# Attention split by queries and its result kept on chip, in a fused attention and feed-forward kernel

## The reference, cut to what matters

```python
# q, k, v: (4, 8, 576, 64), block-causal mask with blocks of 64
scores = q @ k.transpose(0, 1, 3, 2) / sqrt(64)
scores = where(pos_i // 64 >= pos_j // 64, scores, -1e9)
attn = exp(scores - max); attn = attn / (attn.sum(-1) + 1e-9)
x = (attn @ v).transpose(0, 2, 1, 3).reshape(2304, 512)
h = x @ moe_w_in                      # 512 x 2048
g = where(h >= 1, h, where(h <= -1, 0, (h + 1) ** 2 / 4))
x = g @ moe_w_out                     # 2048 x 512
h = x @ moe2_w_in
out = (h * cos(h)) @ moe2_w_out
```

## Time and profile before

| | |
|---|---|
| median of 3 runs | 1106.37 us (1103.53 to 1107.26) |
| span of the profiled execution | 1103.5 us, which is also its time |
| TensorE busy | 1036.5 us, 94% |
| VectorE, ScalarE, POOL busy | 683.7 (62%), 571.5 (52%), 392.7 us (36%) |
| mean granted clock of TensorE | 0.975 |
| first feed-forward matmul | 119.7 us |
| first layer's outputs copied at | 198.9, 272.9, 347.0, 419.6, 492.1, 555.3, 601.4, 647.5 us, ... |
| second layer, one tile | 45.4 us |

### The profile page before, as it was taken

How to read it: one execution, slowest core, us unless ns; L and a number is a source line. 1 busy time by engine, 2 the same in 40 slices (tenths; PEclk the granted TensorE clock), 3 DMA queues, 4 the chain that set the end, 5 groups by cost and what they waited for, 6 DMA issues and landing times.

```text
span 1103.5 us, 21274 instructions
## 1 busy us (share of the span) xinstructions
PE 1036.5 (94%) x7424; PEld 972.7 (88%) x7424; DVE 683.7 (62%) x1308; ACT 571.5 (52%) x1166; POOL 392.7 (36%) x382
## 2 busy tenths in 40 slices
PE   5767899998998999989999999999999999999997
PEld 4646799898998998989999999899999999999996
DVE  6888666767677667676322248755555655556553
ACT  6877565555555655555333236554444444544443
POOL 5877453444353534443221222221222222222221
PEclk8887999999999999999999999999999999999999
DMA  4453212121221121221021025210101101011000
GB/s 152 146 186 125 86 55 71 52 65 65 67 79 56 58 64 61 63 69 41 26 78 38 0 77 176 93 32 7 38 0 38 38 0 38 0 38 38 0 20 20
DMA packets 28513, 64.93 MB, mean 59 GB/s; under 512 B 2880, under 2 KB 11584, under 8 KB 28480
## 3 DMA queue, kind: packets, MB, share of 16 engines
q1 hardware_dynamic: 28480, 64.50, 18.1%
HBM read 50.33 MB, written 14.16 MB: 58 GB/s over the span
## 4 chain that ended last, share of the span: by engine, by line
PE 78%; DVE 9%; ACT 6%; issue 6%; DMA 0%; DVEq 0%; POOL 0%; ACTq 0%; POOLq 0%
PE hidden L1042 35%; PE acc L1061 17%; PE acc L1068 14%; PE heads_out L972 4%; DVE q_parts L699 3%; PE turned L957 2%; PE scores L941 2%; PE scores L942 2%; DVE neg_max L710 2%; ACT probs L495 2%; ACT k_hi L485 1%; ACT q_parts L488 1%; ACT pt_hi L500 1%; DVE pt_lo L726 1%; ACT work L602 1%
## 5 line engine op out<-in xcount | busy, mean ns | idle before, releaser
L441 POOL TENSOR_TENSOR g_lo<-work,g_hi 128x512 fp32r<-128x512 f32 x144 | 189.4, 1315 | 445.6 <-ACT g_hi L608 445.5
L1042 PE MATMUL hidden<-x_hi,win_hi 128*128 128x256 f32 x1152 | 331.0, 287 | 0.8 <-DVE work L849 0.4
L1042 PE MATMUL hidden<-x_lo,win_hi 128*128 128x256 f32 x1152 | 326.9, 284 | 0.0
L1042 PE MATMUL hidden<-x_hi,win_lo 128*128 128x256 f32 x1152 | 325.6, 283 | 0.0
L1042 PEld LDWEIGHTS hidden<-x_hi,win_hi 128*128 128x128 f32 x1152 | 217.7, 189 | 6.0 <-DVE work L849 0.9
L1042 PEld LDWEIGHTS hidden<-x_lo,win_hi 128*128 128x128 f32 x1152 | 218.6, 190 | 2.9
L1042 PEld LDWEIGHTS hidden<-x_hi,win_lo 128*128 128x128 f32 x1152 | 220.1, 191 | 0.0
L399 POOL TENSOR_SCALAR probs<-probs,row_inv 128x512 f32<-128x512 f32 (+4 forms) x130 | 91.2, 708 | 214.2 <-DVE row_inv L722 214.2
L1068 PE MATMUL acc<-g_hi,wout_hi 128*128 128x256 f32 x576 | 166.0, 288 | 0.0
L1068 PE MATMUL acc<-g_hi,wout_lo 128*128 128x256 f32 x576 | 162.3, 282 | 0.0
L1068 PE MATMUL acc<-g_lo,wout_hi 128*128 128x256 f32 x576 | 162.2, 282 | 0.0
(11 more groups left out here) (97 smaller groups left out, 1939.0 us busy)
## 6 DMA issues: line engine op xcount, KB each, us to landing
qk_raw<-qk SPq DMA_DIRECT2D x32, 576.0 KB, 3.7
x_raw<-x_scratch SPq DMA_DIRECT2D x18, 512.0 KB, 3.9
v_raw<-v SPq DMA_DIRECT2D x32, 160.0 KB, 3.5
x_scratch<-out_work SPq DMA_DIRECT2D x32, 144.0 KB, 2.3
x_scratch<-y_stage SPq DMA_DIRECT2D x9, 512.0 KB, 2.7
out<-y_stage SPq DMA_DIRECT2D x9, 512.0 KB, 3.0
x_raw<-w_in SPq DMA_DIRECT2D x8, 512.0 KB, 5.5
y_stage<-w_out SPq DMA_DIRECT2D x8, 512.0 KB, 5.9
```

What stands on the lines that cost most here:

```text
L441: nc.gpsimd.tensor_tensor(g_lo[:, m % G_RING, :], work[:, m % 2, :], g_hi[:, m % G_RING, :], ALU.subtract).then_inc(g_lo_made, 1)
L1042: last = nc.tensor.matmul(into, w[:, p, c, half * P:(half + 1) * P], x[:, c, :], start=(i == 0), stop=(i == len(products) - 1))
```

## The change

A head becomes two items. Items 0 to 31 are the early ones: rows 0 to 255 of a head, two tiles, 256 keys. Items 32 to 63 are the late ones: rows 256 to 575, three tiles, 576 keys. Tokens are reordered so that the early rows of all batches come first: token tile `t` then needs only the first `TILE_ITEMS[t]` items, tile 0 eight of them. Nine early items run alone, with four weight pieces split beside them; the other twelve are split in tile 0 (`weights_beside`), and 264 slots (three per early item, six per late one) are spread over tiles 0 to 6: 24 over 20 units and 9 over 12 in tile 0, 41 over 32 units in tiles 1 to 5, 26 over 20 in tile 6. Sums of the two v parts go straight into a ring of three token tiles on chip (`x_raw`, `X_RING`), `add_parts`; the DRAM scratch and its loads are gone. All attention code is unrolled. ScalarE copies and stores a first-layer tile itself (`store_acc`), and the final output goes out in four DMAs of 64 rows per tile. The padding of narrow matmuls to 192 columns is dropped. Before, k and q came in one load of 576 KB per head; now early items have a load of half the size or less, double-buffered, and late ones one buffer.

```diff
+EARLY, LATE = 256, S - 256
+ITEMS = 2 * HEADS
+SLOTS_OF = (3, 6)
+TILE_ITEMS = [8, 16, 24, 32, 40, 48, 56, 64, 64]
+QUEUE = [(n, k) for n in range(H + 1, ITEMS) for k in range(SLOTS_OF[late(n)])]
+QUEUE += [(ITEMS, k) for k in range(3)]
+PER_TILE = [[(24, 20), (9, 12)]] + [[(41, 32)]] * 5 + [[(26, 20)]]
+WEIGHTS_ALONE = {1: (0, 0), 3: (0, 1), 5: (1, 0), 6: (0, 2)}
...
 # POOL
+            def attention(n, k):
+                if n == ITEMS:
+                    return
+                if k == 0 and not late(n):
+                    split_k(n + 1)
+                if k == 1:
+                    normalise(n, tiles_of(n)[0])
+                    normalise(n, tiles_of(n)[1])
+                if k == 2:
+                    split_v(n)
+                if k == 4:
+                    normalise(n, 4)
+                    if n + 1 < ITEMS:
+                        split_k(n + 1)
...
 # ScalarE
+            def attention(n, k):
                 if k == 0:
+                    if n < ITEMS:
+                        if not late(n):
+                            split_hi(n + 1)
+                        exponential(n, tiles_of(n)[0])
+                        exponential(n, tiles_of(n)[1])
+                    if n:
+                        turned_hi(n - 1, 2 if late(n - 1) else 0)
                 if k == 2:
+                    if n:
+                        move_part(n - 1)
+                    if n < ITEMS:
+                        split_v(n)
+                        if late(n):
+                            turned_hi(n, 0)
                 if k == 3:
                     turned_hi(n, 1)
                     exponential(n, 4)
+                if k == 4 and n + 1 < ITEMS:
+                    split_hi(n + 1)
...
+            def store_acc(t):
                 act.wait_ge(g_used, G_RING + PAIRS * (t + 1))
                 act.wait_ge(y_stored, 16 * (t + 1))
...
                 nc.scalar.activation(y_stage[:, :], acc[:, :, :].rearrange("p a n -> p (a n)"),
                                      ACT.Copy).then_inc(acc_read, 1)
+                act.wait_ge(acc_read, t + 2)
+                nc.scalar.dma_start(x2_dram[t, :, :], y_stage[:, :]).then_inc(y_stored, 16)
...
 # VectorE
+            def attention(n, k):
                 if k == 0:
+                    if n < ITEMS:
+                        row_max(n, tiles_of(n)[0])
+                        row_max(n, tiles_of(n)[1])
+                        if not late(n):
+                            split_q(n + 1)
+                    if n:
+                        turned_lo(n - 1, 2 if late(n - 1) else 0)
+                if k == 1 and n < ITEMS:
+                    inverse(n, tiles_of(n)[0], 2)
                 if k == 2:
+                    if n:
+                        add_parts(n - 1)
+                    if n < ITEMS and late(n):
+                        turned_lo(n, 0)
                 if k == 3:
                     turned_lo(n, 1)
+                    row_max(n, 4)
                 if k == 4:
                     inverse(n, 4)
+                    if n + 1 < ITEMS:
+                        split_q(n + 1)
...
 # TensorE
+            def weigh(n):
+                pe.wait_ge(pt_lo_made, first_turn(n) + (3 if late(n) else 1))
+                pe.wait_ge(v_lo_made, n + 1)
+                if n:
+                    pe.wait_ge(heads_read, n)
+                if late(n):
+                    width = LATE
+                    parts = [(j, LATE * j, max(P * j - EARLY, 0)) for j in range(5)]
+                else:
+                    width = EARLY
+                    parts = [(0, 0, 0), (1, P, P)]
...
             def attention(n, k):
                 if k == 0:
+                    if n < ITEMS:
+                        score(n, tiles_of(n)[0])
+                        score(n, tiles_of(n)[1])
+                    if n:
+                        turn(n - 1, 2 if late(n - 1) else 0)
                 if k == 2:
+                    if n:
+                        weigh(n - 1)
+                    if n < ITEMS and late(n):
+                        turn(n, 0)
                 if k == 3:
                     turn(n, 1)
                     score(n, 4)
```

More of the change, by code:

```diff
@@ L209, in probs_chunk @@
[L209 to L215, removed]
-        def probs_tile(i, alone):
-            whole = probs_chunk(i, alone, 0, EXT[i])
-            return whole.rearrange("p (a n) -> p a n", a=2) if i == QT - 1 else whole
-        def turned_bank(i, alone):
-            return scores[:, 1, :] if alone and i % 2 else turned
@@ L343, in _ @@
-            with sp.Fori(0, 5) as t:
-                beside_tile(t, BESIDE, False)
-            beside_tile(5, HEADS - HEADS_A - BESIDE * 5, True)
+                sp.dma_start(x2_dram[t, :, :], y_stage[:, :]).then_inc(y_stored, 16)
+            load_qk(0)
+            load_first(0, 0)
+            load_v(0)
+            load_qk(1)
+            load_v(1)
+            load_first(1, 0)
+            sp.sem_inc(y_stored, 16)
+            for n in range(ITEMS):
+                after_split(n)
+                for which, pair in FIRST_AFTER.get(n, ()):
+                    load_first(which, pair)
+                if n:
+                    after_split_v(n - 1)
@@ L452, in tile @@
                         hidden_lo(t, s + LAG)
+                    if beside:
+                        for n, k in beside[u]:
+                            attention(n, k)
+                        w = weights_beside(t, u)
+                        if w and w[0] == 1:
+                            split_wout(w[1])
                     s = made_in.get(u)
@@ new lines, in add_parts @@
+            def add_parts(n):
+                dve.wait_ge(part_moved, n + 1)
+                pieces = list(x_pieces(n))
+                for first, cols, place, tile in pieces:
+                    if tile >= X_RING:
+                        dve.wait_ge(x_lo_made, 2 * (tile - X_RING + 1))
+                    last = nc.vector.tensor_tensor(place, heads_out[half_rows(n), first:first + cols],
+                                                   part_sum[half_rows(n), first:first + cols], ALU.add)
+                last.then_inc(heads_read, 1)
@@ L903, in _ @@
             split_q(0)
-            attention_alone(0, True, first=True)
-            with dve.Fori(1, PAIRS) as n:
-                attention_alone(n, True)
-            for n in range(PAIRS, HEADS_A):
-                attention_alone(n, False)
-            split_x(0)
-            end_alone()
+            for n in range(H + 1):
+                for k in range(3):
+                    attention(n, k)
+                w = WEIGHTS_ALONE.get(n)
+                if w and w[0] == 0:
+                    split_win(w[1])
+            split_x(0, False)
             for m in range(LAG):
@@ new lines, in weigh @@
+            def weigh(n):
+                pe.wait_ge(pt_lo_made, first_turn(n) + (3 if late(n) else 1))
+                pe.wait_ge(v_lo_made, n + 1)
+                if n:
+                    pe.wait_ge(heads_read, n)
+                if late(n):
+                    width = LATE
+                    parts = [(j, LATE * j, max(P * j - EARLY, 0)) for j in range(5)]
+                else:
+                    width = EARLY
+                    parts = [(0, 0, 0), (1, P, P)]
+                for j, at, first in parts:
+                    for buf in (pt_hi, pt_lo):
+                        last = nc.tensor.matmul(heads_out[:, first:width], v_parts[:, j, :, :].rearrange("p a d -> p (a d)"),
+                                                buf[:, at + first:at + width], start=(j == 0 and buf is pt_hi),
+                                                stop=(j == parts[-1][0] and buf is pt_lo))
```

848 lines of the change are left out of this document (345 added, 503 removed).

## The result

The changed kernel takes 1265.09 us (median of 4 runs, 1256.34 to 1268.77) where the kernel before takes 1106.82 (1103.53 to 1107.73): 1.143 times as long, 95% interval 1.139 to 1.147. The forecast was slower, 1209 us in a range of 1140 to 1270. The measured time lies in that range, near its upper end.

What follows compares the result with a forecast made beforehand. It took the chain between late items' scores, with TensorE waiting, as the bound: 55 + 8 (lead-in) + 73 + 68 + 464 + 12.5 + 22.7 + 502.1 + 1 = 1206, plus 0.3% gives 1209 us; range 1140 to 1270.

Steps and rivals of the forecast that it cites:

- The alone phase: Attention before any feed-forward work: first hidden matmul at 55 us against 119.7, a gain of 65 us.
- The rival by which TensorE sets the pace (1085): Elementwise engines keep up, late items cost TensorE's own 10.95 us each, total 1085 us; chance 0.11.
- narrow matmuls: 192 unpadded matmuls in attention, taken at 0.11 us each; the upper end adds at most 31 us.
- the term of the late items: Late items beside feed-forward: 32 at 14.5 us, a 14.1 us chain from split_q to split_q plus 0.4, together 464 us.
- the tiles' ends: The x split and store_acc add 2.5 us per tile, 12.5 us together.
- either way the loop's sum differs little: Late items: whether split_q waits for one POOL instruction or more hardly matters, since k_lo is itself the chain's next-to-last link.
- a rival of its own (1240 to 1270, 0.12): TensorE's clock falls in the late stage, adding 1 to 2 us per item: 1240 to 1270 us; chance 0.12.
- a sign that would prove it wrong: A late stage with TensorE's clock under 0.9 would prove the forecast wrong.
- the likeliest case (1150 to 1240): The forecast itself: a late-item loop of 13 to 15.5 us, total 1150 to 1240 us; chance 0.67.
- tile 0: Eleven early items beside feed-forward, eight sharing ScalarE and VectorE with ten weight splits: 73 us.
- tile 1: First 28 units with twelve early items at 5.5 us each, plus 2 for the x split: 68 us.
- the rest of tile 6: After its last slots, 14 units at 20.2 us plus 2.5 for closing turn and weighing: 22.7 us.

Runs made afterwards that it cites:

- e2: Changed kernel with a late item's last score, maximum and exponential moved to slot 2, its inverse, normalise and the next item's splits to slot 3: 1165.66 us.
- e1: Changed kernel with POOL waiting for split_q behind split_k in slot 4: 1255.43 us.
- e13: e4 with turn(n, 1) and its two copies in slot 4 in place of slot 3: 1136.87 us.
- e11: e4 with the output-weight splits beside tile 0 one unit earlier: 1153.57 us.
- b1: The kernel before, with POOL waiting for split_q behind split_k in slot 6: 1086.72 us.
- e7: e4 with turn(n, 1) and its copies one slot later, weigh(n - 1) and move_part(n - 1) one slot earlier: 1197.68 us.
- e9: e4 with SP's wait for v_lo(n - 1) and load of v ahead of tile 0's weight loads: 1154.53 us.
- e3: Changed kernel with split_k(n + 1) ahead of normalise(n, 4) in POOL's slot 4: 1220.49 us.
- e8: e7 with turn(n, 2) and its copies in the item's own slot 5, not the next item's slot 0: 1178.27 us.
- e4: e2 with the next item's splits ahead of the turned copies in slot 3, and e1's wait on POOL: 1152.52 us.

## Why the prediction was right, and where it was off

**Right: the mechanism.** TensorE waits in each late item for the chain that ends in `split_k`, `split_q`. e2 shows it: the same instructions with the chain started a slot earlier give back 99 of the 158 us, or 91 without what lies behind tile 6. The alone phase was forecast at 55 us and took 55.7. TensorE's busy share in tile 3 is 86.97 / 112.1 = 78%, forecast 75. The rival by which TensorE sets the pace (1085) fell with it, and narrow matmuls cost nothing extra, as taken, or a little less.

**Off: the term of the late items**, 32 x 14.5 = 464 with 12.5 for the tiles' ends, 476.5 together. Measured it is 31 x 16.75 from 218.5 to 737.8 and one more, 536: 60 us more, which is about the whole miss (1266.8 against 1206). Two parts of it are shown. First, "either way the loop's sum differs little": it assumed that `split_q` ends 0.35 us behind `k_lo`, but where `hidden_lo` follows directly it waits for that too, 10 us in all (e1). Secondly, the chain was priced at full clock. The item shown above is 17.2 us long, from the end of its `split_q` (389.49) to that of the next one's (406.68), against 14.1 in the forecast's chain, or 14.25 with two units between the slots, as here. Its weighing starts at 395.32, which is 5.8 us in and not 4.4: TensorE has the two score pairs, the turn and two units to do first, at half clock until 393.1. From there to the end of `k_lo` (405.11) the links are as long as forecast to 0.3 us, and 1.3 more come with the third POOL instruction, which 8 of the 32 items have. So the stretch that was too short is the one from the scores to the weighing, with 1.4 of the 2.9 us, and then the last link.

Tiles 2 to 6 ran at 0.85 to 0.90, which the prediction named both as a rival of its own (1240 to 1270, 0.12) and as a sign that would prove it wrong. So the likeliest case (1150 to 1240) did not come; that rival did, by the mechanism it gave. The range held the median by 5 us, because it had been drawn wide enough for that rival and because the gains under "Off the other way" took 13 us back: part of that is luck. Its size: TensorE is busy 1070.8 us in the changed kernel and 1014.8 in e13, with the same matmuls, a difference of 56 us. Of these, 6.9 lie behind tile 6, where both run at 1.00 (485.5 against 478.6), so 49 us of matmul time go with the clock. Not all of that is on the path.

**Off: tile 0**, 90.5 against 73, and tile 1, 83.0, where its first 28 units were put at 68. Late items began at 218.5 us and not at 204, 14 us. The clock is 0.92 and 0.96 there. That output-weight splits delay tile 0 was in the forecast; that the wait for them is 11 us was not, and e11 shows that taking half of it away gives 1.6. What in the tile makes the rest stays open.

**A reading that was off:** the forecast took 1.24 us for `split_q` alone. In the trace each of those eight starts 0.79 us behind the start of a `k_lo` of 1.41 and ends 0.6 behind its end, so it waited for POOL as well, and no row shows it alone. No term of the sum rests on it.

**Off the other way, 13 us:** the rest of tile 6 took 17 us and not 22.7, and tiles 7 to 17 495.2 and not 502.1 with one for the stores. A second-layer tile takes 45.4 us in the kernel before, 44.7 in the profile of the changed one, 43.95 in every experiment on it, and 45.4 again in b1, on the same chip as e7 to e9. So it is not the chip alone. Which part of the change does it was not tried, nor is it known why the changed kernel's own profile stands between: e3 has the same code there and takes 43.95.

**What is left.** e13 is 31 us behind the kernel before, of which its tiles 0 to 6 end 46 us later (647.5 against 601.4) and the rest gives 15 back. Its late item takes 12.75 us against the 10.95 that TensorE would need by my count; at that pace it would take 1137 - 32 x 1.8 = 1079, an estimate. No order that I ran comes there.

## What to carry to other kernels

When attention is cut into more and smaller items, the chain of each is nearly as long as before but has less of the other work beside it: count the chain from one item's scores to the next one's, link by link, before counting any engine's load. A long last link that all wait for (here the splits for the next item) belongs as early in the slots as its inputs allow, and two users of one buffer belong more slots apart than their copies take. And look for cheap instructions on VectorE that overlap several of POOL's: one wait on POOL was worth 1.7% in the kernel before.

## What the runs showed of the hardware

- `split_q` on VectorE takes 0.49 us when it starts 0.07 us ahead of POOL's `normalise` (e8, 465.07), and `normalise` then takes 1.04 in place of 0.74. In the changed kernel the same `split_q`, started behind POOL's, took 3.17 us beside three POOL instructions issued back to back, and ended 0.35 us after the third. The Trainium skill (SBUF — State Buffer, Who interferes with whom) says that the second to issue is blocked until the first is done; here it stayed blocked past the next two as well. With a wait on POOL behind `split_k` the longest was 1.97.
- A POOL instruction that is next in the queue does not always get ahead of the waiting one. In the kernel before, 16 of 21 splits (119 to 600 us) have `split_v` directly behind `split_k` and still run between the two: they take 1.52 us, and `split_v` takes 1.40, against 0.86 beside the others. In e3, where `normalise` stands directly behind `split_k`, `split_q` takes 1.43 in most items and `normalise` 0.98 in place of 0.74 (465.05 and 466.11 us). The five splits of 4.03 us started 0.04 to 0.06 us behind the start of `k_lo`, the sixteen 0.53. What decides which of the two engines gets the next turn no run shows; look at the longest of such a line, not at its median.
- A stop costs TensorE more than its length where the clock falls behind it. Up to the end of tile 6, e3 has 22.8 us less idle time than the changed kernel and 21.0 less busy time; e2 57.3 and 37.7; e13 75.0 and 49.1. In e1, with 11.8 us less idle time, the busy time did not fall at all. The stops for `q_parts` in the changed kernel are 2.9 us on average, 5.2 at the longest. With stops of at most 0.5 us (b1, 268.4 to 407.4 us, two tiles) the granted clock is 1.00. But the tile of the earlier trace rows, with stops of 2.4 and 1.5 us, is at 1.00 too, and the two before it, of the same code, are at 0.98.
- Matmuls of 64 columns step by 0.05 and 0.11 us alternately (e4), cheaper on average than the 0.11 that I took from wider ones.
